# Fused attention and two feed-forward blocks on one core: first queries on two queues, GpSimd's sums regrouped, units 8 to 15 in other slots

## What is computed

```python
# q, k, v: (4, 8, 576, 64)
q_d, k_d, v_d = (t.reshape(B, H, Sd, 4, D).mean(axis=3) for t in (q, k, v))   # pooled by 4
out_up = np.repeat(sm_attn(q_d, k_d, v_d), 4, axis=2)       # softmax attention on 144 tokens
mask = np.abs(pos[:, None] - pos[None, :]) < 4              # local attention, 7 keys a token
out_local = softmax(where(mask, scale * q @ k.T, -1e9)) @ v
x = (out_up + out_local) as (2304, 512)
h = x @ w_in                                                # 512 -> 2048
x = where(h > 0, h, exp(min(h, 0)) - 1) @ w_out             # 2048 -> 512
g = x @ w_gate                                              # 512 -> 1536
x = (g * sigmoid(g) * (x @ w_val)) @ w_out2                 # 1536 -> 512
```

## Time and profile before

| | us |
|---|---|
| median of three runs | 1000.27 (1000.21 to 1001.07) |
| the profiled execution, own time | 999.19 |
| its span, first to last instruction | 997.3 |
| TensorE busy | 985.8 (99%) |
| VectorE, ScalarE, GpSimd busy | 455.7, 341.0, 115.0 |
| mean granted TensorE clock | 0.997 |

### The profile page before, as it was taken

How to read it: one execution, slowest core, us unless ns; L and a number is a source line. 1 busy time by engine, 2 the same in 40 slices (tenths; PEclk the granted TensorE clock), 3 DMA queues, 4 the chain that set the end, 5 groups by cost and what they waited for, 6 DMA issues and landing times.

```text
span 997.3 us, 17826 instructions
## 1 busy us (share of the span) xinstructions
PE 985.8 (99%) x7040; PEld 912.5 (91%) x7040; DVE 455.7 (46%) x1151; ACT 341.0 (34%) x953; POOL 115.0 (12%) x138
## 2 busy tenths in 40 slices
PE   8899999999999999999999999999999999999998
PEld 5889999999999999999999888888888888889997
DVE  7888755556555565564343332223222322322222
ACT  5565544444435344443346321212121221212112
POOL 7204510023000000000057500000000000000000
PEclk9999999999999999999999999999999999999999
DMA  8544521124102111110434300200020001001000
GB/s 241 184 123 106 104 52 43 45 60 100 33 26 77 42 38 33 58 30 1 154 120 131 116 1 1 76 1 1 1 77 1 1 29 47 1 1 39 1 1 37
DMA packets 45666, 55.68 MB, mean 56 GB/s; under 512 B 6504, under 2 KB 33992, under 8 KB 45584
## 3 DMA queue, kind: packets, MB, share of 16 engines
q1 hardware_dynamic: 38128, 50.61, 16.5%
q0 software_dynamic: 6816, 3.55, 2.6%
q10 hardware_dynamic: 640, 0.39, 0.2%
HBM read 45.08 MB, written 9.44 MB: 55 GB/s over the span
## 4 chain that ended last, share of the span: by engine, by line
PE 95%; DVE 2%; ACT 2%; DMA 1%; issue 0%; ACTq 0%; POOL 0%; DVEq 0%; POOLq 0%
PE bank L455 29%; PE bank L457 28%; PE bank L456 28%; PE bank L419 2%; PE bank L386 2%; PE bank L404 1%; PE bank L441 1%; PE bank L395 1%; ACT weights L785 1%; DMA q_first<-qT 1%; DVE weights L616 1%; PE bank L429 0%; ACT prob L746 0%; DVE g_sb L641 0%; ACTq L360 0%
## 5 line engine op out<-in xcount | busy, mean ns | idle before, releaser
L455 PE MATMUL bank<-x_hl,weights 128*128 128x464 f32 (+3 forms) x928 | 325.8, 351 | 4.0 <-DVE weights L616 2.8
L457 PE MATMUL bank<-x_hl,weights 128*128 128x464 f32 (+3 forms) x928 | 322.0, 347 | 0.0
L456 PE MATMUL bank<-x_hl,weights 128*128 128x464 f32 (+3 forms) x928 | 321.9, 347 | 0.0
L455 PEld LDWEIGHTS bank<-x_hl,weights 128*128 128x128 f32 x928 | 175.5, 189 | 15.3 <-DVE weights L616 3.9
L456 PEld LDWEIGHTS bank<-x_hl,weights 128*128 128x128 f32 x928 | 175.6, 189 | 10.2
L457 PEld LDWEIGHTS bank<-x_hl,weights 128*128 128x128 f32 x928 | 175.5, 189 | 10.3
L455 PE MATMUL bank<-g_hl,weights 128*128 128x384 f32 (+1 forms) x448 | 147.7, 330 | 0.0
L457 PE MATMUL bank<-g_hl,weights 128*128 128x384 f32 (+1 forms) x448 | 143.3, 320 | 0.0
L456 PE MATMUL bank<-g_hl,weights 128*128 128x384 f32 (+1 forms) x448 | 143.2, 320 | 0.0
L659 DVE TENSOR_TENSOR u_sb<-bank,u_sb 128x464 f32<-128x464 f32 (+1 forms) x60 | 38.3, 638 | 202.3 <-ACT u_sb L807 202.3
L807 ACT ACTIVATE u_sb<-bank 128x464 f32<-128x464 f32 (+1 forms) x60 | 33.3, 555 | 196.4 <-PE bank L457 196.4
(11 more groups left out here) (96 smaller groups left out, 1062.5 us busy)
## 6 DMA issues: line engine op xcount, KB each, us to landing
landing<-w SPq DMA_DIRECT2D x44, 256.0 KB, 4.0
v_win<-v_windows SPq DMA_DIRECT2D x46, 105.0 KB
q_sb<-qT SPq DMA_DIRECT2D x88, 48.0 KB, 2.3
k_sb<-kT SPq DMA_DIRECT2D x14, 288.0 KB, 3.7
yT_scratch<-y_sb SPq DMA_DIRECT2D x20, 192.0 KB, 2.0
y_raw<-yT_scratch SPq DMA_DIRECT2D x4, 928.0 KB, 5.3
outT<-out_sb SPq DMA_DIRECT2D x16, 232.0 KB, 2.3
landing<-wg SPq DMA_DIRECT2D x12, 256.0 KB, 2.9
```

The costliest lines, as they stand in the source:

```text
L455: nc.tensor.matmul(out, w_hi, x_hi, start=first, stop=False)
L456: nc.tensor.matmul(out, w_hi, x_lo, start=False, stop=False)
L457: return nc.tensor.matmul(out, w_lo, x_hi, start=False, stop=last)
```

## The change

Six edits:

- The half of a unit's first queries for one head is issued by SP, ahead of the unit's keys; the other half stays with ScalarE's queue.
- GpSimd sums the keys of pairs 1, 2 and 3; VectorE those of pair 0 alone.
- GpSimd adds the value rows of pair 0 first. Unit 0 uses that sum, and unit 1 takes the 48 products in its place.
- TensorE: two fillers ahead of the transposes of unit 0 instead of four, five behind instead of three, and the transposes of unit 1 ahead of the outputs of unit 0. ScalarE's copy of unit 1 comes ahead of its first weight piece, and its second weight piece ahead of the copy of unit 3. VectorE's first weight half comes ahead of the output of unit 1.
- The scores of unit 4 (slot 0) stand ahead of the hidden product of step 2 instead of behind it.
- Units 8 to 15 have other slots.

```diff
@@ -85,9 +85,7 @@
 ALIASED = 20
 
-
-ORDER_V = [1, 0, 2, 3]
-SUMMED_BY_PRODUCT = (0, 2, 3)
+SUMMED_BY_PRODUCT = (1, 2, 3)
 
 
@@ -98,7 +96,7 @@
     S_SLOT[_u] = (0, 4, 10, 14)[_u - PROLOGUE]
     NORM_SLOT[_u], T_SLOT[_u], O_SLOT[_u] = S_SLOT[_u] + 3, S_SLOT[_u] + 7, S_SLOT[_u] + 10
 for _u in range(2 * PAIRS, PAIRED):
-    S_SLOT[_u] = 20 + 4 * (_u - 2 * PAIRS)
+    S_SLOT[_u] = (22, 26, 30, 34, 38, 42, 44, 48)[_u - 2 * PAIRS]
     NORM_SLOT[_u], T_SLOT[_u], O_SLOT[_u] = S_SLOT[_u] + 3, S_SLOT[_u] + 5, S_SLOT[_u] + 8
 for _u in range(PAIRED, UNITS):
     S_SLOT[_u] = 56 + 4 * (_u - PAIRED)
@@ -352,12 +350,11 @@
 
 
-        def load_q(eng, u):
+        def load_q(eng, u, half):
             a, p, j = batch_of(u), pair_of(u), third_of(u)
             done = qk_first_loaded[u - 2] if 2 <= u < PROLOGUE else qk_loaded[u % 2]
-            for half in range(2):
-                rows = slice(DH * half, DH * half + DH)
-                eng.dma_start(q_home(u)[rows, half, :], qT[a, p, rows, j * GROUP:(j + 1) * GROUP]).then_inc(done, 16)
+            rows = slice(DH * half, DH * half + DH)
+            eng.dma_start(q_home(u)[rows, half, :], qT[a, p, rows, j * GROUP:(j + 1) * GROUP]).then_inc(done, 16)
 
         def load_k(eng, u):
             a, p, j = batch_of(u), pair_of(u), third_of(u)
@@ -386,10 +383,10 @@
                     nc.tensor.matmul(x[rows, t * WIN:(t + 1) * WIN], q[:, half, t * QT:(t + 1) * QT],
                                      k[:, k0:k0 + WIN], start=True, stop=True)
             pe.wait_ge(q_pooled, u + 1)
-            if a == 0 and p >= 2:
-                pe.wait_ge(k_late_pooled, p - 1)
+            if a == 0 and p > 0:
+                pe.wait_ge(k_late_pooled, p)
             elif j == 0:
-                pe.wait_ge(k_pooled, a * PAIRS + p + 1 if a == 0 else a * PAIRS + p - 1)
+                pe.wait_ge(k_pooled, 1 if a == 0 else (a - 1) * PAIRS + p + 2)
             for half in range(2):
                 rows = slice(DH * half, DH * half + DH)
                 mm = nc.tensor.matmul(x[rows, LOC:SCORES], q_pool[:, u % 2, half, :], k_pool[:, p, :],
@@ -431,7 +428,7 @@
                 mm.then_inc(outputs_done, 1)
                 return
             if a == 0:
-                pe.wait_ge(v_pooled, ORDER_V.index(p) + 1)
+                pe.wait_ge(v_pooled, p + 1)
             else:
                 pe.wait_ge(v_rows_added, 64 * POOL * a)
             for c in range(TILES):
@@ -526,11 +523,11 @@
             pe_filler(pe, 13)
             for u in range(PROLOGUE):
                 pe_scores(pe, u)
-            pe_filler(pe, 4)
+            pe_filler(pe, 2)
             pe_transposes(pe, 0)
-            pe_filler(pe, 3)
+            pe_filler(pe, 5)
+            pe_transposes(pe, 1)
             pe_outputs(pe, 0)
-            pe_transposes(pe, 1)
             pe_transposes(pe, 2)
             pe_outputs(pe, 1)
             pe_transposes(pe, 3)
@@ -541,10 +538,12 @@
             pe_hidden(pe, 1, range(0, 3))
             pe_hidden(pe, 0, range(3, 4))
             pe_hidden(pe, 1, range(3, 4))
+            pe_slot(pe, 0)
             for s in range(STEPS):
                 if s + 2 < STEPS:
                     pe_hidden(pe, s + 2)
-                pe_slot(pe, 2 * s)
+                if s > 0:
+                    pe_slot(pe, 2 * s)
                 pe_accumulate(pe, s)
                 pe_slot(pe, 2 * s + 1)
             pe_gate_val(pe, 0, 0)
@@ -682,7 +681,6 @@
             dve_pool_q(dve, 0)
             dve_pool_k(dve, 0)
             dve_pool_q(dve, 1)
-            dve_pool_k(dve, 1)
             dve.wait_ge(masks_set, 6)
             dve_masked_max(dve, 0)
             dve_pool_q(dve, 2)
@@ -696,8 +694,8 @@
             dve_output(dve, 0)
             dve_normalise(dve, 3)
             dve_x_low(dve, 0)
+            dve_weight_low(dve, 0)
             dve_output(dve, 1)
-            dve_weight_low(dve, 0)
             dve_x_low(dve, 1)
             dve_weight_low(dve, 1)
             dve_output(dve, 2)
@@ -823,7 +821,7 @@
         @block.scalar
         def _(act):
             for u in range(PROLOGUE):
-                load_q(act, u)
+                load_q(act, u, 1)
             act.wait_ge(pool_step, 5)
             for half in range(2):
                 rows = slice(QT * half, QT * half + QT)
@@ -837,13 +835,13 @@
             act_exps(act, 2)
             act_copies(act, 0)
             act_exps(act, 3)
+            act_copies(act, 1)
             act_weight_a(act, 0)
-            act_copies(act, 1)
             act_copies(act, 2)
             act_x_high(act, 0)
+            act_weight_a(act, 1)
             act_copies(act, 3)
             act_x_high(act, 1)
-            act_weight_a(act, 1)
             act_weight_a(act, 2)
             act_x_high(act, 2)
             act_weight_a(act, 3)
@@ -889,17 +887,16 @@
 
         def pool_pool_k(pool, u):
             wait_qk(pool, u)
-            wait(pool, k_late_pooled, u - 2)
+            wait(pool, k_late_pooled, u - 1)
             x = by_token(k_home(u))
             for r in range(2):
                 nc.gpsimd.tensor_tensor(k_halves[:, :, r], x[:, :, r], x[:, :, r + 2], ALU.add).then_inc(k_half_sums, 1)
-            pool.wait_ge(k_half_sums, 2 * (u - 1))
+            pool.wait_ge(k_half_sums, 2 * u)
             nc.gpsimd.tensor_tensor(k_pool[:, pair_of(u), :], k_halves[:, :, 0], k_halves[:, :, 1],
                                     ALU.add).then_inc(k_late_pooled, 1)
 
-        def pool_pool_v(pool, i):
-            p = ORDER_V[i]
+        def pool_pool_v(pool, p):
+
             pool.wait_ge(v_raw_loaded[p], 64)
             if p in SUMMED_BY_PRODUCT:
                 pool.wait_ge(outputs_done, p + 1)
@@ -909,7 +906,7 @@
                     cols = slice(DH * h, DH * h + DH)
                     nc.gpsimd.tensor_tensor(x[:, c, 0:2, cols], x[:, c, 0:2, cols], x[:, c, 2:4, cols], ALU.add).then_inc(v_half_sums, 1)
             pool.wait_ge(zero_rows_set, 3)
-            pool.wait_ge(v_half_sums, 2 * TILES * (i + 1))
+            pool.wait_ge(v_half_sums, 2 * TILES * (p + 1))
             for c in range(TILES):
                 add = nc.gpsimd.tensor_tensor(v_pool[0:PK, 0, p, c, :], x[:, c, 0, :], x[:, c, 1, :], ALU.add)
             add.then_inc(v_pooled, 1)
@@ -946,10 +943,10 @@
             nc.gpsimd.memset(v_win[0:PK, :, :, :], 0.0).then_inc(zero_rows_set, 1)
             nc.gpsimd.memset(v_win_first[0:PK, :, :, :], 0.0).then_inc(zero_rows_set, 1)
             nc.gpsimd.memset(v_pool[:, :, :, :, :], 0.0).then_inc(zero_rows_set, 1)
-            for u in range(2, PROLOGUE):
+            for u in range(1, PROLOGUE):
                 pool_pool_k(pool, u)
-            for i in range(PAIRS):
-                pool_pool_v(pool, i)
+            for p in range(PAIRS):
+                pool_pool_v(pool, p)
             for a in range(1, BATCH):
                 for r in range(POOL):
                     pool_add_rows(pool, a, r)
@@ -960,7 +957,8 @@
 
         def load_qk(sp, u):
             sp.wait_ge(scores_done, u - 3 if u < 6 else u - 1)
-            load_q(sp, u)
+            load_q(sp, u, 0)
+            load_q(sp, u, 1)
             load_k(sp, u)
 
         def load_vwin(sp, u):
@@ -981,7 +979,7 @@
             n = ORDER_A[i]
             wait(sp, w_lo_done, i - LOADS + 1)
             if n >= ALIASED:
-                sp.wait_ge(k_late_pooled, 2)
+                sp.wait_ge(k_late_pooled, 3)
                 sp.wait_ge(v_pooled, PAIRS)
             sp.dma_start(raw(n), w1[n // 2] if n % 2 == 0 else w2[n // 2]).then_inc(piece_loaded[i % LOADS], 16)
 
```

## The result

The changed kernel takes 1005.32 us, the median of five runs (1003.48 to 1006.26), against 1000.21 for five runs of the kernel before, taken in turn with it; the ratio is 1.0051, 95% interval 1.0039 to 1.0063. A second measurement of seven runs gave 1006.60 and 1.0069 (1.0045 to 1.0093). I had forecast 998.8 us and a range up to 1001.0: it is slower, by some 5 us. The profiled execution took 1005.32 itself, with a span of 1003.5, 6.2 more than the span of before.

The account below looks back on a forecast made before the run. TensorE, busy 985.8 of 997.3 us, was taken as the bound, with a ScalarE and VectorE chain setting its last weight wait. 997.3 - 1.7 + 0.25 = 995.85 us span, plus 1.9 and 1.1: 998.8 us, range 997.2 to 1001.0.

Parts of the forecast that it names:

- Units 8 to 15 later: nothing gained: New slots of units 8 to 15: VectorE loses unit work, but TensorE has no wait after 66.87 to give back.
- a loss of 0.25 us: Scores of unit 14 wait for the copy of unit 12's transposes: +0.25 us, bounds 0 and 0.5.
- Term 1, the loads: Prologue loads: one query half per queue lands units 2 and 3 sooner, part of -1.7 us (-1.2 to -2.9).
- bytes, not issues: Prologue loads: units 2 and 3 land as before, leaving only the 0.25 us loss; 1000.5 us, chance 0.17.
- Term 1, TensorE behind it: TensorE to the first hidden bank: outputs, x and weights all 1.7 us earlier, at the same clock as before.
- My clock rival: First hidden products run at 2.4 GHz, VectorE starts on the bank 2.9 us earlier; 997.6 us, chance 0.28.
- The chain's stiffness: ScalarE and VectorE pieces from first hidden bank (28.45) to last weight wait (66.87) move as a block of 38.4 us.
- GpSimd did not become the bound: Prologue rival: GpSimd's key and value sums hold outputs 0; about 1007 us at twice the mean times, chance 0.10.
- a sign of being wrong: TensorE in the prologue: a wait for v_pool was listed among the signs that the forecast is wrong.
- No new weight waits in steps 10 to 13: Steps 10 to 13: new waits for weights were listed among the signs that the forecast is wrong.

Follow-up runs that it names:

- experiment 4: Kernel before with outputs of units 8 to 15 one step later, ten slots behind their scores instead of eight: 1001.89 us, 1.0012 of before.
- the split: Kernel before with only the query halves split over the queues of SP and ScalarE: 999.15 us, 0.9994 of before.
- the order: Changed kernel with the old slot table and both query halves back on ScalarE's queue, leaving the new prologue order: 999.41 us, 0.9999 of before.

## Why the prediction was wrong

- **"Units 8 to 15 later: nothing gained", and a loss of 0.25 us.** This is the step that failed by most. The 0.25 us themselves came true: the copy for unit 12 ran at 117.33, and unit 14's scores started at 117.90 after a wait of 0.25. What the sum left out is 3.7 us by the ruler: the copy of the accumulators behind two slots of attention work at step 15 (1.99), a wait for a copy (0.23), and four small groups standing alone (1.5, this share argued from experiment 4). I had asked of the new table only what units need of each other, not what else stands in ScalarE's order at those steps, nor what a slot shared by two units had saved.
- **Term 1, the loads.** Forecast -1.7 us; the last weight wait came 2.24 later. I took unit 1's keys as issued at 2.35 and landed at about 6.2; they were issued at 2.78, since SP took about 1.3 us a unit and not 1.05, and landed at 7.73. Issuing queries ahead of keys on SP only changed what is late: VectorE began on unit 0 at 5.26 for 5.68, on unit 1 at 7.75 for 7.38. Part of this is chance: in the five profiled executions with the split and GpSimd's sums as before VectorE began on unit 1 between 6.59 and 7.64. The rival "bytes, not issues" came nearest: it had GpSimd's last key sum end at 12.0 (12.21) and unit 2 normalised at 17.4 (17.08). The Trainium skill (DMA: Bandwidth & Descriptors, Issuing engines are not separate DMA queues) says that DMAs of different issuers share 16 engines; here they were 0.97 to 1.03 busy from 6 to 9 us, and the gain of the split at clock 1.000 was 0.5 us. That their load is what made the keys late, no run tells apart from the later issue.
- **Term 1, TensorE behind it.** I kept the clock of before. In the profiled execution outputs of unit 3 took 1.5 us longer (first hidden product 26.22 for 24.19, of which 0.5 was there at 22.65, 0.3 of it from unit 2's slower outputs), and the hidden products up to the bank 0.6. These with the 0.5 make 2.6, less 0.4 in the chain: the 2.24. My clock rival looked at one sign only: up.
- **Right.** The chain's stiffness: 38.1 us; over all profiled kernels 37.4 to 39.5. GpSimd did not become the bound: TensorE's waits for its key sums (0.95, 0.69 and 0.68 us) left VectorE standing for under 0.2 us each, and v_pool was done at 16.6, unit 0's outputs wanted it at 16.90 (in the second profile TensorE did wait for it, 0.33 us, which I had named as a sign of being wrong). No new weight waits in steps 10 to 13. ScalarE's wait for weight pieces (0.58 and 0.81 us) stayed covered.
- **The sum as measured.** At full clock the change without its table is 0.6 us faster than before (one execution; 1.4 with four and three fillers, two executions), the forecast's sign and a third of its size; the table costs 4.0. Of the 5.1 us of the first measurement and the 6.9 of the second that leaves 1.7 and 3.5, which go with the clock: the change's twelve executions run from 1001.38 us at 0.999 to 1009.70 at 0.992. That split and order together bring the long stretches more often than either alone is what the counts say (with thirteen fillers, executions at 0.995 or less: 27 of 46 with both, 6 of 29 with the split, 0 of 11 with the order). Why, no run settled, and before itself went from 7 of 28 to 14 of 30 between two chips.

## What to carry to other kernels

When slots of a hand-written order are moved, list for every engine what else stands at the new places, tile boundaries above all: a copy that frees an accumulator must not stand behind optional work. Put small products next to other small products. Where executions differ in granted clock, compare those at full clock, since an equal mean below it can cost one kernel more than another, or measure from the last wait that belongs to the prologue to the end.

## What the runs showed of the hardware

- The granted clock can fall while TensorE is busy: in the changed kernel TensorE was busy 0.90 to 1.00 in every 1-us stretch from 17 to 23 us, the clock 0.79 in the last of them and 0.50 behind it. The Trainium skill (TensorE: Matmul & The Clock Gate, Part 1) describes a clock that activity releases and that goes back to its lower level after idle time. By the busy share of the profile these rows do not agree: all that stood idle from 17 to 23 us was 0.10 us, between 21 and 22 (0.26 us there in the second profile, in one piece ahead of 21.91).
- One program has executions at 1.000 and at 0.990: before took 998.3 to 1003.0 us over 117 executions, with a median of 998.9 in the 16 at 1.000 and of 1002.3 in the six at 0.991.
- A granted clock of 1.00 does not say that products run at 2.4 GHz: without fillers they stood 0.21 us apart, not 0.11, up to 34.8 us under it.
- Breaking up pairs of small groups of products cost 0.30 us for each pair (seven of them, ruler 2.07 us longer without a wait); 0.18 us of it shows in the spacing of products (0.20 us into and out of the group, 0.11 between full ones).
